# Experts' up projection: weights stationary and tokens moving, byte addresses from one register, a loop unrolled by two

## What is computed

```python
B, S, D, E, F = 4, 576, 512, 8, 1024
logits = x @ w_gate                      # (B, S, E)
for b in range(B):
    for s in range(S):
        e = argmax(logits[b, s]) or prev_e      # a local gate keeps the expert before
        p = softmax(logits[b, s])
        h = np.maximum(x[b, s] @ w1[e], 0.0)    # up: 512 -> 1024
        out[b, s] = p[e] * (h @ w2[e])          # down: 1024 -> 512
```

## Time and profile before

| | |
|---|---|
| median of 3 runs | 989.68 us (989.45 to 989.91) |
| the profiled execution, its own time | 985.62 us |
| its span, first to last instruction | 983.8 us |
| busy share of the span: PE, DVE, ACT, POOL | 94%, 47%, 36%, 29% |
| mean granted clock of TensorE | 0.977 |
| the experts' blocks | from about 672 us to the end of the span |

### The profile page before, as it was taken

One profiled execution on the slowest core, in us unless ns is written; L12 is line 12 of the kernel. 1 busy time (PEld: TensorE's weight loads), 2 busy tenths in 40 slices (PEclk: granted clock), 3 DMA queues, 4 the chain that ended last, 5 costly groups with the idle time before them and its releaser, 6 DMA issues.

```text
span 983.8 us, 20129 instructions
## 1 busy us (share of the span) xinstructions
PE 922.1 (94%) x7739; PEld 584.9 (59%) x7740; DVE 460.1 (47%) x843; ACT 357.5 (36%) x475; POOL 284.6 (29%) x298
## 2 busy tenths in 40 slices
PE   5899999999999999999999999927999999999996
PEld 2566666557676767677767776614555555555552
DVE  4788887664533333333333243668973773000000
ACT  3677776452221212112121112012444444444442
POOL 2477775400110202020201000002443444333331
PEclk9999999999999999999999999968999999999998
DMA  8255542534201011110101102504763672111100
GB/s 284 85 150 157 171 143 67 157 88 150 65 23 44 22 43 35 29 43 21 43 25 39 43 11 83 161 26 123 246 206 124 220 224 80 43 42 50 49 14 1
DMA packets 55340, 89.21 MB, mean 91 GB/s; under 512 B 7140, under 2 KB 26035, under 8 KB 55165
## 3 DMA queue, kind: packets, MB, share of 16 engines
q1 hardware_dynamic: 49853, 72.56, 23.8%
q0 software_dynamic: 5440, 16.00, 5.2%
HBM read 71.19 MB, written 16.55 MB: 89 GB/s over the span
## 4 chain that ended last, share of the span: by engine, by line
PE 85%; DVE 9%; issue 2%; DMA 2%; ACT 1%; SPq 0%; POOL 0%; DVEq 0%; POOLq 0%; ACTq 0%
PE psum L802 19%; PE psum L819 19%; PE psum L978 13%; PE psum L954 13%; PE psum L598 5%; PE psum L741 3%; PE psum L753 2%; PE psum L967 2%; DVE m_mem L1254 2%; DVE arena L1282 2%; PE psum L942 1%; PE psum L619 1%; PE psum L672 1%; PE psum L653 1%; PE psum L763 1%
## 5 line engine op out<-in xcount | busy, mean ns | idle before, releaser
L802 PE MATMUL psum<-m_mem,arena 128*128 (+1 forms) x1728 | 198.8, 273 | 0.3 <-DVE arena L1506 0.3
L819 PE MATMUL psum<-arena,m_mem 128*128 128x512 f16 x864 | 195.3, 379 | 0.0
L802 PEld LDWEIGHTS psum<-m_mem,arena 128*128 128x128 f16 x1728 | 168.4, 98 | 26.1 <-DVE arena L1506 0.7
L819 PEld LDWEIGHTS psum<-arena,m_mem 128*128 128x128 f16 x864 | 84.5, 98 | 90.4
L954 PE MATMUL psum<-arena,m_mem 128*128 x600 | 134.4, 381 | 0.5 <-ACT m_mem L1183 0.5
L1118 ACT ACTIVATE m_mem<-psum 128x512 f16<-128x512 f32 x72 | 43.0, 597 | 251.7 <-PE psum L802 251.7
L978 PE MATMUL psum<-arena,m_mem 128*128 x600 | 133.6, 379 | 0.0
L1414 DVE SCALAR_TENSOR_TENSOR m_mem<-psum,m_mem 128x512 f16<-128x512 f32 x72 | 49.8, 691 | 104.2 <-ACT m_mem L1118 104.2
L954 PEld LDWEIGHTS psum<-arena,m_mem 128*128 128x128 f16 x600 | 58.0, 98 | 65.9 <-issue 1.6
L978 PEld LDWEIGHTS psum<-arena,m_mem 128*128 128x128 f16 x600 | 57.7, 98 | 65.4 <-issue 0.4
L1751 POOL TENSOR_TENSOR arena<-m_mem,arena 128x1024 f16<-128x1024 f32 x9 | 18.0, 1998 | 264.0 <-ACT arena L1133 264.0
(11 more groups left out here) (220 smaller groups left out, 1161.0 us busy)
## 6 DMA issues: line engine op xcount, KB each, us to landing
dimdft_sb<-in_exp_w SPq DMA_DIRECT2D x74, 256.0 KB, 3.2
wstage<-in_exp_w SPq DMA_DIRECT2D x54, 256.0 KB, 3.0
m_mem<-in_qk SPq DMA_DIRECT2D x16, 576.0 KB, 4.5
arena<-in_v SPq DMA_DIRECT2D x32, 160.0 KB, 4.2
x_rows<-m_mem SPq DMA_DIRECT2D x16, 320.0 KB, 3.2
x_rows<-arena SPq DMA_DIRECT2D x9, 512.0 KB, 2.8
wstage<-in_mlp_w SPq DMA_DIRECT2D x16, 256.0 KB, 2.9
arena<-in_mlp_w SPq DMA_DIRECT2D x16, 256.0 KB, 2.8
```

The costliest lines, as they stand in the source:

```text
L802: last = nc.tensor.matmul(psum[:, 2 + k % 4, (f % 2) * 2 * P:(f % 2 + 1) * 2 * P], w1_sb[:, sp_, c, f * P:(f + 1) * P], unT[:, bass.ds(t % ...
L819: last = nc.tensor.matmul(psum[:, 6 + q, :], hT[:, k % 4, sp_, at:at + P], w2_sb[:, mp, f, :], start=f == 0 and sp_ == 0 and mp == 0, stop ...
```

## The change

Three things change in the experts' layer.

First, `up` turns its operands round. A piece of 128 x 128 weights is stationary and the 128 tokens move. Per block that is 8 pieces of hidden columns x 4 slices x 3 products = 96 matmuls of 128 columns. The hidden columns come out in the partitions, which is how `down` wants them. So `transpose_he` and `copy_heT` are gone, with `heT_ready` and `heT_copied`, and `relu` and `he_lo_of` write `heT` themselves. `heT` gets a second copy, used by turns, since block k's hidden values are now written while block k-1's are still to be read by down. New waits: `up` waits for `hs_done` of the block before, `relu` for `he_lo` of the block before and for the down of two blocks before, and `down` for `he_lo` instead of `heT_copied`.

Second, weights are addressed in bytes: `expert_of` keeps the slot's start in bytes in one register, and `slot_part` adds a constant to it for each piece.

Third, PE's loop does two blocks a turn, 11 turns in place of 22, so that the turn (which copy of `heT`) is a constant there. `keep_clock` before the last `down` is gone as well.

```diff
+        slot_bytes = arena[:, :].bitcast(mybir.dt.uint8)
+        def slot_part(slot_at, at, n):
+            return slot_bytes[:, bass.ds(slot_at + 2 * at, 2 * n)].bitcast(F16)
...
-        he_parts = carve([2, FE], F16)
-        heT = carve([2, FE // P, P], F16)
+        heT = carve([2, 2, FE // P, P], F16)
...
-            def up(k, e, slot):
+            def up(k, e, slot, first):
                 pe.wait_ge(xeT_copied, k + 1)
                 pe.wait_ge(w_split, e * ECH + (WCH + ECH))
-                for half in range(2):
+                if not first:
+                    pe.wait_ge(hs_done, k)
+                for f in range(FE // P):
                     for c in range(DC):
-                        for sp_, mp in THREE:
-                            at = mp * EW + c * FE + half * 512
-                            last = nc.tensor.matmul(psum[:, 2 + half, :], xeT[:, sp_, c, :],
-                                                    slots[:, bass.ds(slot, 1), at:at + 512]
-                                                    .rearrange("p o n -> p (o n)"),
+                        for wp, mp in THREE:
+                            last = nc.tensor.matmul(psum[:, 2 + f // 4, f % 4 * P:(f % 4 + 1) * P],
+                                                    slot_part(slot, wp * EW + c * FE + f * P, P), xeT[:, mp, c, :],
...
-            def transpose_he(k):
...
-            def down(k, slot, first=False):
-                pe.wait_ge(heT_copied, k + 1)
+            def down(k, turn, slot, first=False):
+                pe.wait_ge(he_lo, k + 1)
...
-                        at = mp * EW + DC * FE + f * D
-                        last = nc.tensor.matmul(psum[:, 6, :], heT[:, sp_, f, :],
-                                                slots[:, bass.ds(slot, 1), at:at + D]
-                                                .rearrange("p o n -> p (o n)"),
+                        last = nc.tensor.matmul(psum[:, 6, :], heT[:, turn, sp_, f, :],
+                                                slot_part(slot, mp * EW + DC * FE + f * D, D),
...
             def expert_of(k):
                 e = pe.value_load(blkexp[0:1, bass.ds(k, 1)], min_val=0, max_val=E - 1)
-                return e, pe.snap(slot_of(e))
+                return e, pe.snap(slot_of(e) * (2 * SLOT_STEP))
...
-            with pe.Fori(2, NBLK - 1) as k:
-                experts(k)
-            experts(NBLK - 1, last=True)
+            with pe.Fori(2, NBLK - 1, 2) as k:
+                for turn in range(2):
+                    experts(k + turn, turn)
+            experts(NBLK - 1, 0, last=True)
             _, slot = expert_of(NBLK - 1)
-            transpose_he(NBLK - 1)
-            keep_clock(2, 11)
-            down(NBLK - 1, slot)
+            down(NBLK - 1, 0, slot)
...
-            def relu(k):
+            def relu(k, first, early):
                 act.wait_ge(eh_ready, k + 1)
-                nc.scalar.activation(he_parts[:, 0].rearrange("p (b n) -> p b n", b=2), psum[:, 2:4, :], ACT.Relu,
+                if not first:
+                    act.wait_ge(he_lo, k)
+                if not early:
+                    act.wait_ge(blocks_done, k)
+                nc.scalar.activation(heT[:, bass.ds(k % 2, 1), 0].rearrange("p o f s -> p (o f s)"),
...
-            def copy_heT(k):
...
             def he_lo_of(k):
                 pool.wait_ge(hs_done, k + 1)
-                nc.gpsimd.tensor_tensor(he_parts[:, 1], hs, he_parts[:, 0], ALU.subtract).then_inc(he_lo, 1)
+                part = [heT[:, bass.ds(k % 2, 1), i].rearrange("p o f s -> p (o f s)") for i in range(2)]
+                nc.gpsimd.tensor_tensor(part[1], hs, part[0], ALU.subtract).then_inc(he_lo, 1)
```

More of the change, by code:

```diff
@@ L436, in fused_kernel @@
         hs_done = sem("hs_done")
-        heT_ready = sem("heT_ready")
         he_hi = sem("he_hi")
         he_lo = sem("he_lo")
-        heT_copied = sem("heT_copied")
         blocks_done = sem("blocks_done")
@@ L944, in transpose_xe @@
                 last.then_inc(xeT_ready, 1)
-            def up(k, e, slot):
+            def up(k, e, slot, first):
                 pe.wait_ge(xeT_copied, k + 1)
                 pe.wait_ge(w_split, e * ECH + (WCH + ECH))
-                for half in range(2):
+                if not first:
+                    pe.wait_ge(hs_done, k)
+                for f in range(FE // P):
                     for c in range(DC):
-                        for sp_, mp in THREE:
-                            at = mp * EW + c * FE + half * 512
-                            last = nc.tensor.matmul(psum[:, 2 + half, :], xeT[:, sp_, c, :],
-                                                    slots[:, bass.ds(slot, 1), at:at + 512]
-                                                    .rearrange("p o n -> p (o n)"),
-                                                    start=c == 0 and sp_ == 0 and mp == 0,
-                                                    stop=c == DC - 1 and sp_ == 1)
+                        for wp, mp in THREE:
+                            last = nc.tensor.matmul(psum[:, 2 + f // 4, f % 4 * P:(f % 4 + 1) * P],
+                                                    slot_part(slot, wp * EW + c * FE + f * P, P), xeT[:, mp, c, :],
+                                                    start=c == 0 and wp == 0 and mp == 0,
+                                                    stop=c == DC - 1 and wp == 1)
                 last.then_inc(eh_ready, 1)
-            def transpose_he(k):
+            def down(k, turn, slot, first=False):
                 pe.wait_ge(he_lo, k + 1)
[L964 to L969, removed]
-            def down(k, slot, first=False):
-                pe.wait_ge(heT_copied, k + 1)
                 if not first:
@@ L986, in expert_of, with experts @@
                 e = pe.value_load(blkexp[0:1, bass.ds(k, 1)], min_val=0, max_val=E - 1)
-                return e, pe.snap(slot_of(e))
-            def experts(k, first=False, last=False, second=False):
+                return e, pe.snap(slot_of(e) * (2 * SLOT_STEP))
+            def experts(k, turn, first=False, last=False, second=False):
                 e, slot = expert_of(k)
@@ L992, in experts @@
                     _, last_slot = expert_of(k - 1)
-                    transpose_he(k - 1)
-                up(k, e, slot)
+                up(k, e, slot, first)
                 if not last:
@@ L997, in experts @@
                 if not first:
-                    down(k - 1, last_slot, second)
+                    down(k - 1, 1 - turn, last_slot, second)
             keep_clock(4, 12)
@@ L1003, in _ @@
             slots_second()
-            experts(0, first=True)
-            experts(1, second=True)
-            with pe.Fori(2, NBLK - 1) as k:
-                experts(k)
-            experts(NBLK - 1, last=True)
+            assert NBLK % 2 == 1
+            experts(0, 0, first=True)
+            experts(1, 1, second=True)
+            with pe.Fori(2, NBLK - 1, 2) as k:
+                for turn in range(2):
+                    experts(k + turn, turn)
+            experts(NBLK - 1, 0, last=True)
             _, slot = expert_of(NBLK - 1)
-            transpose_he(NBLK - 1)
-            keep_clock(2, 11)
-            down(NBLK - 1, slot)
+            down(NBLK - 1, 0, slot)
         @block.scalar
@@ L1184, in copy_xeT @@
                     .then_inc(xeT_copied, 1)
-            def relu(k):
+            def relu(k, first, early):
                 act.wait_ge(eh_ready, k + 1)
-                nc.scalar.activation(he_parts[:, 0].rearrange("p (b n) -> p b n", b=2), psum[:, 2:4, :], ACT.Relu,
+                if not first:
[3 more added lines that the diff above has]
+                nc.scalar.activation(heT[:, bass.ds(k % 2, 1), 0].rearrange("p o f s -> p (o f s)"),
+                                     psum[:, 2:4, :].rearrange("p b n -> p (b n)"), ACT.Relu,
                                      scale=1.0 / WS).then_inc(he_hi, 1)
-                nc.scalar.activation(hs.rearrange("p (b n) -> p b n", b=2), psum[:, 2:4, :], ACT.Relu, scale=1.0 / WS)\
+                nc.scalar.activation(hs, psum[:, 2:4, :].rearrange("p b n -> p (b n)"), ACT.Relu, scale=1.0 / WS)\
                     .then_inc(hs_done, 1)
-            def copy_heT(k):
[L1195 to L1199, removed]
             def weigh(k, first):
@@ L1210, in experts @@
             def experts(k, first=False, second=False, last=False):
-                if not first:
-                    copy_heT(k - 1)
-                relu(k)
+                relu(k, first, first or second)
                 if not last:
@@ L1224, in _ @@
             experts(NBLK - 1, last=True)
-            copy_heT(NBLK - 1)
             weigh(NBLK - 1, False)
```

## The result

| | before | after |
|---|---|---|
| median of the compared runs, us | 989.68 (988.45 to 991.27, 7 runs) | 994.51 (992.12 to 996.25, 7 runs) |
| ratio, 95% interval | | 1.0044 (1.0032 to 1.0056) |
| the profiled execution, its span, us | 985.6, 983.8 | 992.1, 990.3 |
| mean granted clock | 0.977 | 0.978 |
| from the start of up(0) to the end of up(1), us | 17.11 | 18.76 |

The changed kernel is slower by 0.44%, 4.8 us, and the forecast of 993.7 us for a slower kernel holds. The profiled executions were quicker than the medians, by 4.1 us before and 2.4 after, so their spans differ by 6.5 us and not by 4.8.

A forecast was written before the change was run, and what follows sets the result against it. PE bounds the kernel; after the change its sequencer (period 11.9 us) outlasts the array (10.97). Terms +4.6 + 1.6 - 2.2 = +4.0 us give 989.6 profiled; with the median 4.1 above, 993.7 us, range 979 to 1003.

The forecast's parts named there:

- The array's side: PE's array per block: up 5.34 us instead of 5.18, hidden-row transposes gone (-0.89), total 10.97 us, 0.73 less than before.
- The turnaround of an addition: PE's sequencer between up's and down's matmuls: 115 ns per address addition, 78 a block, 8.97 us.
- rival 1: Sequencer between matmuls: additions hand over faster; chance 0.28 of gaining over 2 us (middle 980), 0.18 no change (0.111 to 0.114).
- The head, the entries: Sequencer per block: expert-number loads with assertions, mean 1.65 us (1.9 or 1.4); entering up 0.3, down 0.1.
- The sequencer now needs more than the array's 10.97, so it sets the period: PE, each block: sequencer work 11.80 us plus 0.1 to 0.2 lost to a full queue, period 11.9 us.
- 23 periods: From the end of up(1) to the end of up(24): each period 0.2 us longer, +4.6 us.
- The beginning: Up(0) and up(1), each 7.45 us at the sequencer's pace; up(1) ends at 692.65 instead of 691.10, +1.6 us.
- The end: After the last up: down(24) starts at 966.6 instead of 968.80, following the weighing of down(23), -2.2 us.
- The sum: Whole kernel: +4.6 + 1.6 - 2.2 = +4.0 us, 989.6 in the profiled execution, forecast median 993.7.
- 2 (98 ns a load): Up on the array: 96 weight loads in a row don't hide; up 9.4 us, block 15.0, time 1066; chance 0.03.
- 3 (half clock): PE's array, fed with gaps, gets the lower clock; a block about 22 us, some 1235 in all; chance 0.02.
- The page's rule against the change: Up on the array at about 81 ns a matmul: 7.8 us, a block 13.4, the estimate 39 us more.

The follow-up runs named there:

- e1: Changed kernel with up multiplying by the fixed identity matrix instead of the expert's weights, so up needs no addresses; 970.32 us, ratio 0.98.
- e2: Changed kernel with the old slot-index addresses, a fused address instruction for each weight piece in up and down; 1012.77 us, ratio 1.0235.
- e4: Changed kernel with the slot of the block before kept in a register instead of loaded and worked out again; 991.06 us, ratio 1.0011.
- e5: Changed kernel with the last four of up's eight pieces multiplying by the identity, so without addresses; 972.9 us, ratio 0.9829.
- e6: Changed kernel with the first four of up's eight pieces multiplying by the identity, so without addresses; 975.22 us, ratio 0.9865.

## Why the prediction was right, and where it was not

- **What bounds the kernel: right.** PE is the chain; the copies removed from ACT were worth nothing (ACT waits up to 5.6 us a block for PE).
- **The array's side: right.** Up 5.34 predicted, 5.41 in e1; the array's floor 10.97 predicted, 11.04 to 11.06 measured, 970.3 us in all.
- **The turnaround of an addition: right**, 115 ns taken and 116 measured in the mean. Most steps are 112 to 113 ns, which alone would have been rival 1's strip around no change; about every eighth is 142 to 143. The mean of 129 for the fused form, from which the 115 was worked out, holds such long steps too (124 ns mostly, 154 at times), so this is no luck. It was the term on which the sign hung, and e2 shows its weight: 11 ns more made 18 us.
- **The head, the entries: right in size.** The head without a branch was taken at 1.4 us; from its first instruction (899.07 us) to the addition behind its second assertion (900.50) it is 1.43.
- **"The sequencer now needs more than the array's 10.97, so it sets the period": right for this kernel, and not a rule.** The prediction put the sequencer's work at 11.80 us and the time in which the full queue stops it at "about 0.1 to 0.2 lost". The trace has no stop in the block with the branch (11.97 us, all of it the sequencer's own work) and 0.42 us in the block without (11.83). So the work is 11.7 in the mean and the stop 0.2: both terms came out. What the prediction did not say is that the second term is no constant. Shorten the head, and the stop grows by nearly as much (e4: 0.10 us gained of 0.7). Once the queue is full when up starts, another account holds: down 5.18, token transposes 0.52, and up from its own start (96 - 17) x 0.077 = 6.1, together 11.8. That covers the blocks without the branch here and all of e4. Where the queue never fills, the sum holds as it stands: in the blocks with the branch here, and in e2. For this kernel the two accounts lie within 0.2 us of each other; only experiments could tell them apart.
- **23 periods: +5.03 against +4.6.** 23 x 0.22 = 5.0. Mean period 11.92 against 11.9 predicted.
- **The beginning: +1.65 against +1.6**, though up(1) came by another way. The timeline of PE after:

```profile
675.59 7.80 PE L958 MATMUL psum<-m_mem,arena 128*128 128x128 f16 x96 [0.43 <-ACT m_mem L1173]
683.23 0.61 PE L945 MATMUL psum<-identb_sb,m_mem 128*128 128x128 f16 x8
686.69 7.82 PE L958 MATMUL psum<-m_mem,arena 128*128 128x128 f16 x96 [2.85 <-ACT m_mem L1173]
694.35 0.61 PE L945 MATMUL psum<-identb_sb,m_mem 128*128 128x128 f16 x8
```

  Up(0) took 7.64 us and up(1) 7.66 (7.45 predicted), the gap between them is what the relu passes and the token copy take. In up(1) the granted clock is low again, after the idle 2.85 us before it:

```profile
687.00:690.00 3.00, 3.00 (x31) 2.98 (x31) 2.93 (x5) 0.00 (x0) 2.16 (x3) 0.51 0.39 109
```

  (stretch; its length, busy PE, PEld, DVE, ACT, POOL; clock, DMA share, GB/s.) While the clock is low, the array starts a pair each 107 ns, slower than the sequencer's 77, so the queue fills meanwhile, and the next 30 or so pairs start 56 ns apart. The half clock cost this up nothing next to up(0) at full clock. In the kernel before it cost up(1) 0.8 us (5.97 against 5.18).
- **The end: -1.8 against -2.2.** Down(23) ends with the chain's L970, the weighing follows (974.18), and down(24) starts at 975.16, 6.5 us after up(24)'s end instead of 6.2. The last up is also longer than those before it, 6.39 us against 6.13 and 6.26. What leaving out `keep_clock` is worth by itself, no run shows.
- **The sum: +4.0 forecast, +4.9 measured.** The two profiled spans differ by 6.5 us, of which 4.9 lie in the experts (1.65 + 5.03 - 1.78) and 1.6 ahead of them, where the kernels are the same: that part is chance between two executions. The medians differ by 4.8.
- **The rivals.** 1 (a faster addition) falls by its measured mean of 116 ns. 2 (98 ns a load) falls by e1. 3 (half clock) falls: the granted clock is 1.00 from 692 us to 972.
- **The page's rule against the change.** The Trainium skill, "TensorE: Matmul & The Clock Gate", section "Back-to-back issue gap", gives about 81 ns for a matmul of 128 columns in such a stream. e1 measures 56 ns over 96 in a row, so the page's figure doesn't hold for the array here. The 75 to 77 ns of up's later part is near it, but is made by two address additions for three matmuls, and goes away with them.

## What to carry to other kernels

Count two clocks for a stream of matmuls: the array, and the sequencer with its addresses (here 112 to 116 ns for each new register address among matmuls, whatever the matmul's size). Cutting moving columns from 512 to 128 leaves the array's time and multiplies the addresses per microsecond; the page shows such an engine as fully busy, so look at the starts of loads and address instructions in two stretches of one pass. With a queue of limited depth the sum of the sequencer's work decides only as long as the queue doesn't fill; once it does, what counts is where in the order address-poor work stands. Mixing address-poor matmuls into address-rich ones, with no work saved, gave back 5 us here (6 on top of the shorter head), and a shorter loop head then took 0.23 us off the period instead of 0.10.

## What the runs showed of the hardware that was not expected

- The lead of the sequencer over the array was 17 load-and-matmul pairs wherever a full queue let it be counted, under matmuls of 216 ns and under matmuls of 56 ns (e5, e6) alike. So it counts pairs, not time: 3.7 us of cover in the one case, 0.95 in the other.
- Additions between matmuls start 112 to 113 ns apart, and about every eighth 142 to 143, though each is listed at 32 ns. The fused form, 14 ns longer by its own duration (46), is 11 ns longer from start to start (127 against 116).
- In the later part of an up of the kernel after, each third weight load starts 112 to 113 ns after the one before it, the other two 55 to 58. The granted clock stayed at 1.00 over these ups (700 to 972 us); an idle time of 2.85 us was followed by 0.51.
- A stretch at half clock cost a stream paced by addresses nothing: up(0) at full clock and up(1), with 0.51 for 3 us of it, took 7.64 and 7.66 us.
